# Loading each expert's first matrix in four 512 KB blocks instead of two of 1 MB, each with its own semaphore

## The reference

```python
# attention over buckets: 8 heads, 768 tokens, head size 64
scores = np.where(q_bucket == k_bucket, scale * q @ k.T, -1e9)
x = softmax(scores) @ v                      # reshaped to 768 x 512
# mixture of experts: E = 8, capacity 192, w1 512 x 1024, w2 1024 x 512
expert_idx = np.argmax(x @ w_gate, axis=1)   # one expert for each token
h = np.maximum(np.einsum('ecd,edf->ecf', disp, w1), 0.0)
y = np.einsum('ecf,efd->ecd', h, w2)
out[i] = gate_w[i] * y[expert_idx[i], pos[i]]
# last layer: w_in 512 x 2048, w_out 2048 x 512
g = h * np.tanh(log1p(exp(h)))
return g @ w_out
```

## Time and profile before

| | us |
|---|---|
| median of 3 runs | 397.11 |
| lowest and highest | 396.93, 397.86 |
| the profiled execution: its own time | 397.2 |
| the profiled execution: span | 395.4 |
| TensorE busy in the span | 383.8 |
| expert stage | about 142.4 to 257.9 |

### The profile page before, as it was taken

One profiled execution on the slowest core, in us unless ns is written; L12 is line 12 of the kernel. 1 busy time (PEld: TensorE's weight loads), 2 busy tenths in 40 slices (PEclk: granted clock), 3 DMA queues, 4 the chain that ended last, 5 costly groups with the idle time before them and its releaser, 6 DMA issues.

```text
span 395.4 us, 6819 instructions
## 1 busy us (share of the span) xinstructions
PE 383.8 (97%) x2386; PEld 346.2 (88%) x2388; DVE 283.6 (72%) x446; ACT 234.1 (59%) x448; POOL 118.8 (30%) x122
## 2 busy tenths in 40 slices
PE   8989999999999999899999999999999999999995
PEld 3678999999999798889997998899899988999984
DVE  4788898889998645540446745669899998877861
ACT  5969869969887434530435653457666666544531
POOL 0863642742820060039645325500000000000015
PEclk9999999999999999999999999999999999999999
DMA  8593944984910047996899999190000000000004
GB/s 281 211 218 88 269 101 102 309 164 95 403 64 0 4 161 281 383 342 220 309 338 385 319 392 372 58 301 19 2 0 2 0 0 2 0 0 2 0 5 159
DMA packets 16956, 62.89 MB, mean 159 GB/s; under 512 B 3088, under 2 KB 3984, under 8 KB 12448
## 3 DMA queue, kind: packets, MB, share of 16 engines
q1 hardware_dynamic: 15424, 58.61, 44.4%
q0 software_dynamic: 992, 3.19, 2.2%
q10 hardware_dynamic: 512, 0.73, 0.6%
HBM read 49.89 MB, written 3.19 MB: 134 GB/s over the span
## 4 chain that ended last, share of the span: by engine, by line
PE 58%; DMA 4%; POOL 1%; issue 1%; POOLq 0%; ACT 0%; DVE 0%; SPq 0%; ACTq 0%
PE ps L1064 17%; PE ps L1089 16%; PE ps L939 13%; PE ps L984 9%; DMA ring<-in_w 2%; PE ps L1005 2%; DMA rows<-xg,sloti 1%; PE ps L965 1%; POOL rows L646 0%; POOLq L102 0%; POOL out L667 0%; DVE outs L1710 0%; ACT yh L1282 0%; ACT ysb L1276 0%; SPq L500 0%
## 5 line engine op out<-in xcount | busy, mean ns | idle before, releaser
L939 PE MATMUL ps<-xs,ring 128*128 x512 | 60.9, 277 | 1.2 <-DMA ring<-in_w 1.2
L939 PEld LDWEIGHTS ps<-xs,ring 128*128 128x128 f32 x512 | 59.3, 191 | 2.5 <-issue 2.1
L1517 DVE TENSOR_TENSOR ptl<-ps,pth 128x384 fp32r<-128x384 f32 x96 | 48.9, 551 | 4.4 <-ACT pth L1217 3.8
L1217 ACT ACTIVATE pth<-ps 128x384 fp32r<-128x384 f32 x96 | 42.0, 490 | 16.0 <-PE ps L861 15.1
L1440 DVE TENSOR_REDUCE nmax<-ps 128x1 f32<-128x768 f32 x48 | 45.7, 955 | 5.8 <-PE ps L731 3.4
L731 PE MATMUL ps<-ops 128*128 128x384 f32 x192 | 44.4, 353 | 1.6 <-ACT ops L1138 0.9
L1171 ACT ACTIVATE prob<-ps,nmax 128x768 f32<-128x768 f32 x48 | 43.5, 906 | 0.1
L1064 PE MATMUL ps<-yh,wih 128*128 128x384 f32 x128 | 43.0, 336 | 0.3 <-ACT yh L1282 0.3
L1064 PE MATMUL ps<-yh,wlow 128*128 128x384 f32 x128 | 42.8, 335 | 0.0
L1606 DVE TENSOR_TENSOR w2lo<-ring,w2hi 128x1024 fp32r<-128x1024 f32 x28 | 38.7, 1383 | 5.6 <-ACT w2hi L1272 5.6
L1064 PE MATMUL ps<-yl,wih 128*128 128x384 f32 x128 | 42.0, 335 | 0.0
(11 more groups left out here) (193 smaller groups left out, 785.1 us busy)
## 6 DMA issues: line engine op xcount, KB each, us to landing
ring<-in_w SPq DMA_DIRECT2D x32, 1024.0 KB, 6.7
wraw<-in_w_in SPq DMA_DIRECT2D x11, 256.0 KB, 5.8
wraw<-in_w_out SPq DMA_DIRECT2D x11, 256.0 KB, 6.1
ops<-kh SPq DMA_DIRECT2D x12, 192.0 KB, 6.3
ops<-qh SPq DMA_DIRECT2D x6, 384.0 KB, 8.4
xg<-rows SPq DMA_DIRECT2D x1, 1539.0 KB, 6.2
raw<-in_vt SPq DMA_DIRECT2D x4, 384.0 KB, 5.5
wraw<-in_w_in SPq DMA_DIRECT2D x1, 1280.0 KB, 11.1
```

The costliest lines, as they stand in the source:

```text
L939: last = mm(ps[:, fc // 2, (fc % 2) * WIDE:(fc % 2) * WIDE + W], wa[:, 2 * fc // KF, kd, P * (fc % (KF // 2)):P * (fc % (KF // 2)) + P], x ...
L1217: av(pth[:, (n // HT) % 2, HT * b:HT * b + HT, n % HT, :], ps[:, tile_banks(n)[b], 0:HALF].rearrange("p (a c) -> p a c", c=P), ACT.Copy).t ...
L1517: V.tensor_tensor(ptl[:, m2, HT * b:HT * b + HT, u, :], ps[:, tile_banks(n)[b], 0:HALF].rearrange("p (a c) -> p a c", c=P), pth[:, m2, HT ...
```

## The change

The first matrix is cut into four blocks of 256 columns instead of two of 512. On the host it is laid out so that a block is contiguous; a partition's part of a block is 4 KB instead of 8 KB. SyncE issues four loads of 512 KB with a semaphore each, each after its own count of `Hw`, and TensorE waits for a block ahead of every second `fc`.

```diff
-        wa = ring[0][:, :].rearrange("p (h c n) -> p h c n", h=2, n=F // 2)
+        wa = ring[0][:, :].rearrange("p (h c n) -> p h c n", h=4, n=F // 4)
...
-            def first_weights(e, half):
-                sp.dma_start(wa[:, half, :, :], w1[bass.ds(e, 1), half, :, :, :].rearrange(
-                    "o p c n -> (o p) c n")).then_inc(s[f"wa{half}"], 16)
+            def first_weights(e, part):
+                sp.dma_start(wa[:, part, :, :], w1[bass.ds(e, 1), part, :, :, :].rearrange(
+                    "o p c n -> (o p) c n")).then_inc(s[f"wa{part}"], 16)
...
-                for half in range(2):
-                    if g == 1:
-                        first_weights(0, half)
-                    elif g == 2:
+                if g == 1:
+                    for part in range(4):
+                        first_weights(0, part)
+                elif g == 2:
+                    for half in range(2):
                         second_weights(0, half)
...
-                for half in range(2):
-                    hold(sp, s["passed_sp"], s["Hw"], 4 * i + 2 * half + 2)
-                    first_weights(i + 1, half)
+                for part in range(4):
+                    hold(sp, s["passed_sp"], s["Hw"], 4 * i + part + 1)
+                    first_weights(i + 1, part)
...
-                        if fc % (KF // 2) == 0:
-                            pe.wait_ge(s[f"wa{2 * fc // KF}"], 16 * (e + 1))
+                        if fc % 2 == 0:
+                            pe.wait_ge(s[f"wa{fc // 2}"], 16 * (e + 1))
...
-                                      wa[:, 2 * fc // KF, kd, P * (fc % (KF // 2)):P * (fc % (KF // 2)) + P],
+                                      wa[:, fc // 2, kd, P * (fc % 2):P * (fc % 2) + P],
...
-              "w1": w1.reshape(E, DM // P, P, 2, F // 2).transpose(0, 3, 2, 1, 4),
+              "w1": w1.reshape(E, DM // P, P, 4, F // 4).transpose(0, 3, 2, 1, 4),
```

More of the change, by code:

```diff
@@ L75, in attention_moe_mish @@
     E, _, _, KD, F = w1.shape
-    DM, F = KD * P, 2 * F
+    DM, F = KD * P, 4 * F
     FF = w_in.shape[1] * P
@@ L256, in attention_moe_mish @@
         sems = {}
-        for n in ["first_" + n for n in MISH_A + MISH_B] + ["wm" + str(f) for f in [*range(BEFORE, NS), *range(NS, KFF, 2)]] + ["still", "c0", "c", "cr", "k0", "q00", "q01", "k1", "q1", "pj", "pj2", "qs", "cl", "passed_sp", "passed_gp", "rk0", "rk1", "rv0", "rv1", "ca", "cq", "cp", "pja", "pjb", "ah", "ab", "ao", "ak", "aq", "ka", "kl", "ks", "ch", "cc", "opsA", "opsB", "wa0", "wa1", "wb0", "wb1", "wi", "wo", "out",
+        for n in ["first_" + n for n in MISH_A + MISH_B] + ["wm" + str(f) for f in [*range(BEFORE, NS), *range(NS, KFF, 2)]] + ["still", "c0", "c", "cr", "k0", "q00", "q01", "k1", "q1", "pj", "pj2", "qs", "cl", "passed_sp", "passed_gp", "rk0", "rk1", "rv0", "rv1", "ca", "cq", "cp", "pja", "pjb", "ah", "ab", "ao", "ak", "aq", "ka", "kl", "ks", "ch", "cc", "opsA", "opsB", "wa0", "wa1", "wa2", "wa3", "wb0", "wb1", "wi", "wo", "out",
                   "pjh", "pjl", "wg",
```

## The result

The changed kernel takes 398.65 us (median of 22 runs) and the kernel before 397.29 (median of 22): ratio 1.0033, 95% interval 1.0023 to 1.0042. By the ratio that is 1.3 us slower, where I had forecast 0.6 us faster, and above the end of my range, 397.9. The profiled execution of the changed kernel has a span of 397.3 us, 1.9 more than that of before.

The account below looks back on a forecast made before the run. TensorE, busy 383.8 of 395.4 us, was taken as the bound, its stands hanging on late `wb0`. Terms +0.2 - 0.6 - 0.2 - 0.2 + 0.2 = -0.6 us gave 396.5 us, range 395.7 to 397.9.

Parts of the forecast that it names:

- The bound: Narrow experts: late `wb0` delays ScalarE, then VectorE, then TensorE at `fc` = 4; 1.82 us to regain in all.
- The waits on TensorE and the issues on SyncE: Two more products with a wait (at most 0.16 us) and two more issues (0.83 us, covered): put at nothing.
- The packets: Loads of `wa`: 4 KB rows instead of 8 KB cost 0.2 us per first matrix, bounds nothing to 0.54.
- Expert 1: All of `wa` still ahead of `wb0`, with 0.2 us more in packets: +0.2 us (0 to +0.54).
- Expert 4: Earlier blocks let `wb0` land near 206.3, so TensorE's stand at `fc` = 4 goes: -0.6 us (0 to -0.6).
- The slower start of expert 5: The slower start behind expert 4's late quarters would go: -0.2 us (0 to -0.2).
- experts 6 and 7: `wb0` landing 0.5 us earlier in expert 6 would remove expert 7's slower start: -0.2 us (0 to -0.2).
- my own signs: Profile marks set beforehand, among them expert 4: ScalarE's wait under 0.4 us, about 13.1 us in all; wrong if `wb0` takes 6.6.
- The open microsecond: DMA engines 0.92 busy from 194 to 201, leaving 0.56 us open that earlier issues can fill.
- What comes late next: Last layer's blocks land earlier, so GpSimd's splits lie beside more of VectorE's quarters: +0.2 us (0 to +0.4).
- The rule: Batch DMAs to 1 MiB or more; by its fit four blocks take 12.8 us instead of 8.8, expert 1 losing 4.
- the rival that took up that rule: Every load has a price in a full queue, ahead of `wb0` in expert 1: +2.0 at 1 us each, 399.1; chance 0.13.

Follow-up runs that it names:

- Loosening that link: First half of the second matrix (`wb0`) in two loads of 512 KB, ScalarE waiting for each: 0.9982 on the kernel before, 0.9972 on the changed kernel.
- second trace of the changed kernel: The changed kernel run once more, unedited, beside another set of runs of the kernel before: 397.76 us, ratio 1.0023.

## Why the prediction was wrong

*The bound* was read rightly. `wb0`, ScalarE, VectorE, TensorE at `fc` = 4 is the path in the changed kernel too. VectorE ends the third quarter of expert 4 at 212.07 + 1.60 = 213.67, and TensorE goes on at 214.50, 0.83 us later; I had read 0.84. Loosening that link made both kernels faster, the changed one clearly, the kernel before by 0.0018 with an interval that just reaches 1.

*The waits on TensorE and the issues on SyncE* I put at nothing. The kernel with all of them and the old times is at 0.9998, and its interval ends at 1.0017, so together they cost at most 0.7 us and most likely nothing.

*The packets* I put at 0.2 us. Two loads with 4 KB rows measure 0.999, no loss that could be told from none, though 0.2 us is too little for that run to see. From 157 to 164 us, with the new rows in the full queue, the changed kernel moves 424 GB/s against 425 before, which leaves nothing of the term there.

*Expert 1*, +0.2 us: the second layer went on 0.05 us later. But its loads were issued 0.42 us earlier than before (152.69 against 153.11), so `wb0` took 12.35 us where it took 11.9; in this trace the term is about 0.45 us, inside its bounds. Over the eight traces that have four blocks and `wb0` in one load it is 11.8 to 12.4 us, 12.1 in the mean, so 0.2 was a fair size, but the packets, for which I had put it, are not shown to be its cause. That the stage was 0.42 us ahead at that point was luck for the total; no run gives a reason. As I had said, the earlier start of the first layer was lost again at `fc` = 4, though it was larger than the 0.1 us I gave it.

*Expert 4*, -0.6 us, is the step that failed. I took the landing of `wb0` as a matter of the bytes left in the queue, 0.56 us of open time filled and 1.25 us less work ahead of it, so blocks out of the way earlier could only help. Half of the engines did as the sum says, 1.0 us earlier than before; the load landed 0.7 us later, with its last engine. The term measured +0.65 instead of -0.6, and I had no case in which an earlier issue does harm. The slower start of expert 5, -0.2, came out as +0.24, and experts 6 and 7, for which I had -0.2 more, as +0.90 and +0.07, by the same step. Of my own signs three said so: ScalarE's wait in expert 4 was 1.77 us and not under 0.4, expert 4 took 14.30 us and not 13.1, and its `wb0` landed 7.3 us after its issue, beyond the 6.6 that I had named as a sign of being wrong. What stands in its place: a load is as late as its last engine, and that depends on when the loads ahead of it are issued, not on their bytes alone. The runs show this for the timing as a whole; the reason for the late engine stays open.

*The open microsecond* was real. I counted 0.56 us of open queue from 194 to 201 as a gain to be had. The earlier issues filled it (a share of 1.02 and 404 GB/s from 194 to 201, where it was 0.92 and 302), and from 201 to 203 1.3 us worth of bytes went missing in its stead, 0.8 us of it idle: the work had only been moved away from the point where the next load starts. Before, the same two us moved 623 KB, not 291.

*What comes late next*, +0.2 us for GpSimd's splits beside VectorE: they started later, not earlier, since their loads are behind `wb`. VectorE's third quarter of expert 4 took 1.60 us, as before.

*The range.* Its upper end was added up wrongly: 397.1 + 0.54 + 0.4 is 398.0, not 397.9. The measured time is above both.

*The rule.* The Trainium skill, page "DMA: Bandwidth & Descriptors", section "Bandwidth", says to batch loads to 1 MiB or more. Its measured table, like its fit, is for loads issued from GpSimd; those here are issued from SyncE. The direction came true for this change, but not by its mechanism: four loads of 512 KB at the old times cost nothing, and at better times they are 0.3% faster than two of 1 MB. The case is not evidence for a fixed price of a load in a full queue, and so the rival that took up that rule, 399.1, falls too, though its time was the nearest.

## What to carry to other kernels

When a buffer is refilled piece by piece, the times of the pieces decide how soon the load behind them lands, and issuing each as early as it comes free is not always best. Here the best was to issue the first half early and 1 MB at the last count (0.9976 and 0.9969); 1 MB there with the first half late was like before (0.9998), 512 KB there was worse or no better (1.0033, 1.0023, 1.0001), and 2 MB was worst (1.0071). Since the reason is not shown, try the times rather than carry the sizes over. Look for the one load on which the chain hangs and judge each edit by its landing: of the pieces of `wa` none was ever waited for in experts 3 to 7, in any of these traces but that with 64 partitions, and their timing moved the kernel from 0.997 to 1.007.

## What the hardware showed that I had not expected

The same load of 1 MB, `wb0` of expert 4, took 7.3 us in the changed kernel, where the last block ahead of it was done 5.6 us before it landed, against 6.6 before with twice the bytes at the last count, and 5.3 in the best version; a lone one took 4.8. In the second trace of the changed kernel it was 6.4. Of the sixteen engines' reports fifteen came within 0.5 us of each other and the last one 2.4 us later (expert 4: 205.1 to 205.6, then 208.0). And with the first matrix in loads of 64 partitions the DMA engines had a share of 1.01 at 289 GB/s, where with 128 partitions it went with 425.
